# Attention on one NeuronCore: which operand of the product of probabilities and values stands in the TensorE array, and who sums the probabilities

## The reference, cut to what matters

```python
mask = q_bucket[:, :, :, None] == k_bucket[:, :, None, :]
scores = scale * np.matmul(q, k.transpose(0, 1, 3, 2))
scores = np.where(mask, scores, -1000000000.0)
scores = scores - np.max(scores, axis=-1, keepdims=True)
attn = np.exp(scores)
attn = attn / (np.sum(attn, axis=-1, keepdims=True) + 1e-09)
return np.matmul(attn, v).astype(np.float32)
```

## Time and profile before

| what | value |
|---|---|
| median of three runs | 567.22 us (566.21 to 567.86) |
| profiled execution, its time | 567.58 us |
| profiled execution, span of the core | 565.8 us |
| mean granted TensorE clock | 0.972 |
| TensorE matmul busy | 491.5 us (87%), 2706 records |
| TensorE weight loads busy | 311.3 us (55%), 2706 |
| VectorE busy | 324.2 us (57%), 532 |
| ScalarE busy | 314.1 us (56%), 469 |
| GpSimd busy | 126.3 us (22%), 83 |
| chain that ended last, by engine | PE 68%, DVE 10%, DMA 7%, issue 6%, ACT 6%, POOL 1% |

### The profile page before, as it was taken

One profiled execution on the slowest core, in us unless ns is written; L12 is line 12 of the kernel. 1 busy time (PEld: TensorE's weight loads), 2 busy tenths in 40 slices (PEclk: granted clock), 3 DMA queues, 4 the chain that ended last, 5 costly groups with the idle time before them and its releaser, 6 DMA issues.

```text
span 565.8 us, 7554 instructions
## 1 busy us (share of the span) xinstructions
PE 491.5 (87%) x2706; PEld 311.3 (55%) x2706; DVE 324.2 (57%) x532; ACT 314.1 (56%) x469; POOL 126.3 (22%) x83
## 2 busy tenths in 40 slices
PE   4589999999999999999986776677698889998996
PEld 3455565555555565555543222123387668886874
DVE  4246546565455655555555311016999897888850
ACT  2376876667866667776755100002744775676650
POOL 3134030030302103000000000005333455454641
PEclk9999999999999999999999796789999999999999
DMA  8888454696537963270009499993000020001001
GB/s 195 191 165 193 94 132 86 162 320 144 116 71 188 316 137 76 57 247 1 0 9 393 194 376 394 375 372 118 0 0 1 0 75 1 2 0 74 0 0 74
DMA packets 49330, 75.69 MB, mean 134 GB/s; under 512 B 24752, under 2 KB 27696, under 8 KB 48688
## 3 DMA queue, kind: packets, MB, share of 16 engines
q1 hardware_dynamic: 48792, 73.85, 44.7%
q10 hardware_dynamic: 504, 1.39, 1.1%
HBM read 51.45 MB, written 3.15 MB: 96 GB/s over the span
## 4 chain that ended last, share of the span: by engine, by line
PE 68%; DVE 10%; DMA 7%; issue 6%; ACT 6%; POOL 1%; ACTq 0%; DVEq 0%; POOLq 0%
PE unit L282 32%; PE o_acc L282 22%; PE unit L892 13%; DMA w<-in_moe_w 6%; ACT turned L534 3%; DVE nmax L677 2%; DVE fu L802 2%; DVE g L813 1%; DVE fe L797 1%; ACT probs L526 1%; PE unit L954 1%; DMA op<-bit 1%; POOL g_lo L500 1%; ACT fe L614 1%; DMA turned<-in_q 1%
## 5 line engine op out<-in xcount | busy, mean ns | idle before, releaser
L677 DVE TENSOR_REDUCE nmax<-unit 128x1 f32<-128x768 f32 x96 | 91.9, 957 | 107.2 <-PE unit L282 107.1
L526 ACT ACTIVATE probs<-unit,shift,keep 128x768 f32<-128x768 f32 x96 | 95.2, 991 | 81.1 <-DVE shift L680 79.3
L282 PE MATMUL unit<-op 128*128 128x512 f32 (+1 forms) x384 | 93.3, 366 | 9.1 <-DMA op<-bit 6.2
L892 PEld LDWEIGHTS unit<-ident,probs 128*128 128x128 f32 x576 | 62.4, 142 | 58.0 <-ACT probs L526 42.9
L500 POOL TENSOR_TENSOR g_lo<-g,g_hi 128x1024 fp32r<-128x1024 f32 x24 | 73.0, 3041 | 88.4 <-ACT g_hi L621 88.4
L892 PE MATMUL unit<-ident,probs 128*128 128x128 f32 x576 | 85.0, 285 | 2.0 <-ACT probs L526 2.0
L282 PE MATMUL o_acc<-turned,vn 128*64 128x384 f32 x384 | 82.7, 511 | 0.1
L534 ACT COPY turned<-unit 128x768 f32<-128x768 f32 x96 | 76.2, 793 | 2.0 <-PE unit L892 2.0
L282 PEld LDWEIGHTS unit<-op 128*128 128x128 f32 x384 | 60.1, 195 | 21.5 <-issue 6.6
L282 PE MATMUL unit<-wo_hi,g_hi 128*128 128x512 f32 x96 | 38.9, 405 | 12.4 <-DVE m_pack L791 5.5
L813 DVE TENSOR_TENSOR g<-fv,fr 128x1024 f32<-128x1024 f32 x24 | 45.9, 1911 | 3.8 <-ACT fr L630 3.8
(11 more groups left out here) (116 smaller groups left out, 629.6 us busy)
## 6 DMA issues: line engine op xcount, KB each, us to landing
w<-in_moe_w SPq DMA_DIRECT2D x16, 2048.0 KB, 12.0
op<-cuts SPq DMA_DIRECT2D x31, 384.0 KB
op<-cuts SPq DMA_DIRECT2D x31, 192.0 KB
w_in_sb<-in_moe_w_in SPq DMA_DIRECT2D x1, 4096.0 KB, 19.5
wo_raw<-in_moe_w_out SPq DMA_DIRECT2D x2, 2048.0 KB, 16.8
vn<-in_v SPq DMA_DIRECT2D x8, 384.0 KB, 3.4
out_x<-stage SPq DMA_DIRECT2D x12, 256.0 KB, 2.4
qn<-in_q SPq DMA_DIRECT2D x14, 192.0 KB, 4.5
```

What stands on the lines that cost most here:

```text
L282: return nc.tensor.matmul(out_, lhsT, rhs, start=start, stop=stop, skip_group_check=True)
L526: sc.activation(probs[i % 3][:, :], unit("S", i)[:, 0:S], ACT.Exp, bias=shift[:, g % 4, t:t + 1], scale=keep[:, g % 4, t:t + 1], accum_out ...
L677: ve.tensor_reduce(nm, unit("S", i)[:, 0:S], AX.X, ALU.max, negate=True).then_inc(max_done, 1)
L892: ins = nc.tensor.transpose(u[:, f], probs[i % 3][:, f], ident[:, :])
```

## The change

The turned probabilities of one tile (128 keys x 128 queries) now stand in the array, six times in turn for the six key blocks, and the values run through. The values lie in rows of 65, with a column of ones as the 65th, so the product's 65th column is the sum of the probabilities. The result has the queries on the partitions and needs no turning back: `copy_out`, `turn_out`, the F units and `halves` are gone, and VectorE normalises straight from the bank. ScalarE's exponential no longer has `accum_out`. `turned` has three buffers of one tile. A product follows each slot (`weigh(i - 1)`) in place of the thirds.

The two banks of `o_acc` belong to one head each in turn. The bank that rests takes the preparation of the next pair: the queries and keys are turned in four pieces of 3 transposes, in slots 2 to 5 of an odd head (`side_piece`), and the hash stands in slot 2 of an even head. Each load of values is now two DMAs, one per head, into rows of 65. GpSimd writes the ones in two memsets before the program starts on its constant rows.

The core of the diff:

```diff
+    def side_piece(h, s):
+        pair = h // 2 + 1 if h % 2 == 0 else (h + 3) // 2
+        if pair >= NP or s < 2:
+            return None
+        if h % 2 == 1:
+            return "T", 4 + 4 * (pair - 2) + s - 2
+        return ("H", pair) if s == 2 else None
...
-        vn = [sb(f"vn{n}", [P, 2, T, D]) for n in range(2)]
+        vn = [sb(f"vn{n}", [P, 2, T, D + 1]) for n in range(2)]
-        turned = [sb(f"turned{n}", [P, T, 3, P]) for n in range(2)]
+        turned = [sb(f"turned{n}", [P, T, P]) for n in range(3)]
+        def o_bank(g):
+            return o_acc[:, 512 * (g % 2):512 * (g % 2) + 512]
+        def rest_bank(h):
+            return o_bank(h + 1)
...
-                sp.dma_start(vn[n % 2][:, :, :, :], v_h[:, 2 * n:2 * n + 2, :, :]).then_inc(v_in[n % 2], 16)
+                for h in range(2):
+                    sp.dma_start(vn[n % 2][:, h, :, 0:D], v_h[:, 2 * n + h, :, :]).then_inc(v_in[n % 2], 16)
...
+            for n in range(2):
+                link(gp.memset(vn[n][:, :, :, D:D + 1].rearrange("p h t d -> p (h t) d"), 1.0))
+            pool.sem_inc(ones_set, 1)
...
-                              scale=keep[:, g % 4, t:t + 1], accum_out=sums[:, g % 4, t:t + 1]).then_inc(exp_done, 1)
+                              scale=keep[:, g % 4, t:t + 1]).then_inc(exp_done, 1)
...
+                copy_probs(i)
+                piece = side_piece(h, s)
+                if piece and piece[0] == "T":
+                    copy_turned_half(h, piece[1])
+                if i + LEAD < T * G:
+                    exponentials(i + LEAD)
...
+            def norm(g):
+                mixed = o_bank(g)[:, 0:T * (D + 1)].rearrange("p (t d) -> p t d", t=T)
+                dve.wait_ge(pv_done, T * (g + 1))
+                ve.tensor_scalar(den[:, :], mixed[:, :, D], EPS, 0.0, ALU.add, ALU.add).then_inc(den_done, 1)
+                ve.reciprocal(rden[:, :], den[:, :]).then_inc(rden_done, 1)
+                ve.tensor_tensor(x_cols(g), mixed[:, :, 0:D],
+                                 rden[:, :].unsqueeze(2).broadcast_to([P, T, D]), ALU.mult).then_inc(normed, 1)
...
-                for e in range(2):
-                    t = 2 * j + e
-                    ins = mm(bank[D * e:D * e + D, :], vn[g // 2 % 2][:, g % 2, t, :],
-                             turned[half % 2][:, t, :, :].rearrange("p n q -> p (n q)"), j == 0, j == 2)
+                for k in range(T):
+                    ins = mm(o_bank(g)[:, (D + 1) * t:(D + 1) * (t + 1)], turned[i % 3][:, k, :], vn[g // 2 % 2][:, g % 2, k, :],
+                             k == 0, k == T - 1)
                 ins.then_inc(pv_done, 1)
...
+                turn_probs(i)
+                piece = side_piece(h, s)
+                if piece and piece[0] == "T":
+                    turn_half(h, piece[1])
+                if piece and piece[0] == "H":
+                    if h > 0:
+                        pe.wait_ge(normed, h)
+                    hashes(piece[1], rest_bank(h))
+                if i + LEAD < T * G:
+                    scores(i + LEAD)
+                if i >= 1:
+                    weigh(i - 1)
+            weigh(T * G - 1)
```

More of the change, by code:

```diff
@@ L124, in build_program @@
         bit = sb("bit", [P, HS], F32R)
[L125 removed]
+        vn = [sb(f"vn{n}", [P, 2, T, D + 1]) for n in range(2)]
         probs = [sb(f"probs{n}", [P, S], at=e_at if n < 2 else None) for n in range(3)]
[L128 to L132 removed]
+        turned = [sb(f"turned{n}", [P, T, P]) for n in range(3)]
+        first_qk = [t[:, :, :].rearrange("p k q -> p (k q)").rearrange("p (h t d) -> p h t d", h=2, t=T)
+                    for t in turned[0:2]]
         hash_w = sb("hash_w", [P, 32])
@@ L526, in exponentials @@
                 sc.activation(probs[i % 3][:, :], unit("S", i)[:, 0:S], ACT.Exp, bias=shift[:, g % 4, t:t + 1],
-                              scale=keep[:, g % 4, t:t + 1], accum_out=sums[:, g % 4, t:t + 1]).then_inc(exp_done, 1)
+                              scale=keep[:, g % 4, t:t + 1]).then_inc(exp_done, 1)
             def copy_probs(i):
                 act.wait_ge(p_turned, i + 1)
[L532 to L551, removed]
+                if i >= 3:
+                    act.wait_ge(pv_done, i - 2)
+                sc.copy(turned[i % 3][:, :, :].rearrange("p k q -> p (k q)"), unit("P", i)[:, 0:S]).then_inc(p_by_act, 1)
             act.dma_start(first_qk[1], k_h[:, 0:2, :, :]).then_inc(k_in, 16)
@@ L649, in link, with bits @@
                 dve.wait_ge(dve_chain, chain[0])
-            def bits(n):
+            def bits(n, hashes):
                 dve.wait_ge(hashed, n + 1)
@@ L680, in row_max @@
                 ve.tensor_scalar(shift[:, g % 4, t:t + 1], nm, -MASKED, nm, ALU.is_lt, ALU.mult).then_inc(shifted, 1)
[L682 to L689, removed]
-                    dve.wait_ge(normed, g)
[L691 to L708, removed]
+            def norm(g):
+                mixed = o_bank(g)[:, 0:T * (D + 1)].rearrange("p (t d) -> p t d", t=T)
+                dve.wait_ge(pv_done, T * (g + 1))
+                if g >= 1:
+                    dve.wait_ge(rden_done, g)
+                ve.tensor_scalar(den[:, :], mixed[:, :, D], EPS, 0.0, ALU.add, ALU.add).then_inc(den_done, 1)
+                dve.wait_ge(den_done, g + 1)
+                if g >= 1:
+                    dve.wait_ge(normed, g)
+                ve.reciprocal(rden[:, :], den[:, :]).then_inc(rden_done, 1)
+                dve.wait_ge(rden_done, g + 1)
+                ve.tensor_tensor(x_cols(g), mixed[:, :, 0:D],
+                                 rden[:, :].unsqueeze(2).broadcast_to([P, T, D]), ALU.mult).then_inc(normed, 1)
             for cols in (slice(QB, KB + 1, 2), slice(QA, KA + 1, 2)):
@@ L717, in _ @@
             cut_low_first(1)
-            for kind, i in UNITS:
-                in_order(kind, i)
+            bits(0, unit("H", 0))
+            for i in range(LEAD):
+                row_max(i)
+            for h, s in SLOTS:
+                piece = side_piece(h, s)
+                if piece and piece[0] == "H":
+                    bits(piece[1], rest_bank(h))
+                if T * h + s + LEAD < T * G:
+                    row_max(T * h + s + LEAD)
+                if s == 0 and h > 0:
+                    norm(h - 1)
+            norm(G - 1)
             link(ve.tensor_reduce(sel4[:, :], ident[:, :].rearrange("p (g s) -> p s g", g=4), AX.X, ALU.add))
@@ L911, in turn_out @@
[L911 to L930, removed]
@@ L935, in _ @@
+            pe.wait_ge(consts, 1)
+            turn(0)
+            turn(1)
+            u = claim("H", 0)
+            pe.wait_ge(proj_in, 32)
+            hashes(0, u)
+            turn(2)
+            turn(3)
+            for i in range(LEAD):
+                scores(i)
             for h, s in SLOTS:
                 i = T * h + s
[L937 to L944, removed]
+                turn_probs(i)
+                piece = side_piece(h, s)
+                if piece and piece[0] == "T":
+                    turn_half(h, piece[1])
+                if piece and piece[0] == "H":
+                    if h > 0:
+                        pe.wait_ge(normed, h)
+                    hashes(piece[1], rest_bank(h))
+                if i + LEAD < T * G:
+                    scores(i + LEAD)
```

93 lines of the change are left out of this document (45 added, 48 removed).

## The result

The changed kernel took 571.8 us (median of 20 runs, 568.39 to 574.82), the kernel before 567.05 us on the same chips: a ratio of 1.0076, 95% interval 1.0056 to 1.0096. It is slower by 0.8%; forecast were 570.2 us and 0.5%. The profiled execution took 572.66 us, its span is 570.9 us and its mean granted clock 0.954.

The account below looks back on a forecast made before the run. TensorE was taken to set the pace. Terms +35.5 - 27.0 - 5.2 + 1.0 - 1.3 = +3.0 us on 567.58 gave 570.6, or 570.2 us against the runs' median; own range 565 to 575, 8 in 10 within 557 to 582.

Parts of the forecast that it names:

- +3.0: Sum of all terms, in us, against the profiled execution's 567.58 us, giving 570.6 us.
- The price of a load: New product of probabilities and values: 0.111 us per load, 12 loads or 1.33 us a tile, +35.5 us in all.
- The faster pace of P: Rival: the product's loads keep the 0.100 us of the probabilities' turning, 557.5 us; chance 0.25, shared with 107 ns.
- 107 ns: Rival: the product's loads take columns divided by 1.2, in ns, 564.8 us; chance 0.25, shared with the 0.100 us pace.
- S and the gaps: Scores on TensorE take 0.70 us for 0.87; gaps into and out of the product go; slot 2.66 us against 2.30.
- Load and stream: In the new product, 65 columns of stream, 0.055 us, lie beneath the load of 0.111 us, which sets the pace.
- The rival from the Trainium skill: The product's loads and streams run one behind the other, 0.166 us a record, 63 us more: 633 us; chance 0.03.
- T, H and the tail: Query/key transposes in pieces -5.2 us; hash paying its own gap +1.0; attention's end, 2.43 us shortened to 1.1, -1.3.
- F: Turning the product back on TensorE goes: 15 times 1.80 us, -27.0; the sixteenth is counted in the tail.
- The values at the start: First pair's values, needed three slots earlier and loaded by two DMAs: between 0 and 1.5 us, taken as 0.
- what stands behind that wait on TensorE: At the start: if the first values are late, the turning of slot 2's probabilities stands behind the product on TensorE.
- the clock is at its upper level in every slice of the attention: Kernel before, attention up to 295 us: granted clock at 2.4 GHz in every slice.

Follow-up runs that it names:

- c2: The changed kernel with the first values issued in front of the second head's spread: 566.79 us, 0.9998 of the kernel before.
- d2: The changed kernel with each matmul of the product made of two, for 64 queries each, on the array's two column halves: 541.97 us, 0.9535 of the kernel before.
- d1: The changed kernel with five of six matmuls of each product streaming 33 of 65 columns, loads unchanged: 572.67 us, 1.0095 of the kernel before.
- d3: The kernel before without the product's copy, the turning back and the sum of halves, normalising one bank: 541.85 us against 566.94, 0.9563.
- f2: The changed kernel with five of six matmuls of each product made of two 64-column loads, both on the same array half: 602.93 us, 1.0638 of the kernel before.
- c1: The changed kernel as it is, measured again for comparison on one chip: 572.4 us, 1.0112 of the kernel before.
- g1: d2 again, values loaded as in the changed kernel, on the same chip as g2: 541.92 us, 0.956 of the kernel before.
- c3: The changed kernel with 27 transposes of the identity in front of the wait for the first values: 570.83 us, 1.0081 of the kernel before.
- c4: c2 with the product in fp32r, 576 loads in place of 1152: 514.27 us, 0.9073 of the kernel before.
- g2: g1 with the first values issued early, on the same chip: 539.2 us, 0.9511 of the kernel before.

## Why the prediction was right

It was right in direction and, within 1.6 us, in size. Two errors of it cancelled in part, so that closeness is in part luck: the start cost 5.6 us where it had 0, and the rest came out about 2.6 us cheaper than its +3.0 (by the medians, c2 lies 0.4 us above the kernel before).

- *The price of a load*: 0.111 us forecast, 0.112 measured inside the group. The faster pace of P, and the Trainium skill's 107 ns, did not come for the loads inside the group. From one group to the next, though, W takes 1.28 in place of 1.33.
- *S and the gaps*: measured by its loads, S takes 0.70, and the gap into W is gone, as said. The slot is 2.65 for 2.66. d2 brought the gap back by bringing the halves back. What the prediction did not see is the other side of the split. It read the halves as the source of the gaps only, and not as two streams at once; its sum was not hurt, as it took W's 0.80 from a row.
- *Load and stream*: d1 shows that the stream lies beneath the load. The rival from the Trainium skill (TensorE: Matmul & The Clock Gate, The mechanism) falls for loads of the whole array: they are loaded ahead of the stream though every one uses all rows, at 0.112 us a record, where one behind the other would be 0.166.
- *T, H and the tail*: 0.31 a piece for 0.33; 0.95 for H behind P (1.54 - 0.59) for 0.79 + 0.16; the tail 1.08 for 1.1 (296.06 + 2.79 to 299.93).
- *F*: 1.80 a place forecast, 1.83 in the slots of d3's profile that have no H. With the tail in it the forecast was 28.3 (27.0 + 1.3); d3's median gives 25.1 and its profiled execution 28.3 (567.58 - 539.28).
- *The values at the start*: this step failed. The text said "Between 0 and 1.5 us, TensorE being idle about there anyway; I take 0", and c2 shows 5.6 us. The first load was issued at 25.4 us as before, but as two DMAs one behind the other, and by the chain of waits the values landed at about 30.8. The rows that I went by did not have that time of issue. With the median of 3.2 us to landing it gives 29.2 already for the first of the two, and TensorE wanted the values at about 27.9 (an estimate from the S that starts at 27.07). I had named what stands behind that wait on TensorE, but had bounded its cost by 1.5 us. The clock that falls behind it was left out. The prediction said that the clock is at its upper level in every slice of the attention; that was the page's digit, and the pace of the groups before 29 us speaks against it.
- *The sum without it*: c2 turns its output at 294.5 us, where my +3.0 on the 295.08 of before gives 298.1. Of the 3.6 us, 96 slots x 0.01 are 1.0. Some 1.8 lie in the first three slots, where I had counted two products at full price. c2 takes 9.11 us for them (24.26 to 33.37) and the kernel before 8.38 (23.94 to 32.32), only 0.7 more with two products of 1.28 in them. The kernel before idled there for ScalarE, 0.26 and 0.58 us, and was at half pace until about 29 us, where c2 was at full clock from 27.4 on. The 0.8 left are smaller differences. This part is read from the traces and was not tried by itself.

So the main parts nearly cancel, as the sum said (35 us more for the product, 33 less for what it makes superfluous), and by c2 they cancel wholly. The 5 to 6 us by which the changed kernel is slower come from its first values, which were not loaded early enough.

## What to carry to other kernels

When operands change places, count the columns that are loaded and not only those that stream: with 128 columns standing and 65 or fewer running, an fp32 matmul here costs its two loads, 0.22 us. When a group moves earlier in the order, follow its first input back to the issue of its DMA; behind a wait of TensorE stands everything, and the clock may fall as well. And before a split of the array is given up, see whether its halves work at once: a product whose output splits by 64 rows can load and stream both halves side by side, and here that was worth 30 us.

## What the runs showed of the hardware that I had not expected

- Matmuls whose outputs lie on the two halves of 64 rows, issued in turn, start within 0.01 us of each other, and so do their loads (d2, and W in the kernel before). From pair to pair pass 0.06 us, so 128 columns are loaded in that time in place of 0.112. On one half a load of 64 columns takes 0.058, and two of them bring nothing (f2).
- Waits of TensorE for the values early in the attention (1.66 us in c1, 2.09 in g1, 2.92 in the changed kernel's first profile, 4.59 in d2) were each followed by a stretch at 1.2 GHz, and in c3, with work in the wait, there was none.
- A wait of 1.08 us at the end of the attention was followed by 1.2 GHz in four profiles (the changed kernel, c3, c4, d1) and not in others (c1, c2, d2, g1, g2).
- The page's clock line can read 9 where the matmuls run at half pace: in the kernel before, until about 29 us.
